# Two units pulled ahead of the first pairs, eight staging places, a table in six transfers, and a last tile that is written by tokens

## The reference, cut to what matters

```python
X = np.fft.rfft(x, axis=1)                       # x: 4 x 3008 x 256
Yr, Yi = Xr @ w_r - Xi @ w_i + b_r, Xr @ w_i + Xi @ w_r + b_i
Yr = np.sign(Yr) * np.maximum(np.abs(Yr) - 0.01, 0.0)   # Yi likewise
y = np.fft.irfft(Yr + 1j * Yi, n=3008, axis=1)
h = y.reshape(12032, 256) @ w_in                 # 256 x 2048
g = np.maximum(h, 0.0) + alpha * np.minimum(h, 0.0)
out = g @ w_out                                  # 2048 x 256
```

## Time and profile before

| | |
|---|---|
| median of 3 runs | 1375.19 us (1373.89 to 1375.62) |
| the profiled execution | 1378.68 us, of which the span is 1376.9 us |
| PE busy | 1360.3 us of the span (99%) |
| PEld, DVE, ACT, POOL busy | 84%, 75%, 55%, 24% |
| granted clock over the whole span | 0.996 |

### The profile page before, as it was taken

The page is one execution under the profiler, slowest core; times in us unless marked ns, Lnnn a source line. Parts: engine busy times, 40 slices in busy tenths (PEclk is TensorE's granted clock), DMA queues, the critical chain, the costliest instruction groups (busy, mean ns, idle before and its releaser), DMA issues.

```text
span 1376.9 us, 21744 instructions
## 1 busy us (share of the span) xinstructions
PE 1360.3 (99%) x6933; PEld 1158.1 (84%) x6933; DVE 1026.8 (75%) x1892; ACT 763.7 (55%) x1711; POOL 327.9 (24%) x370
## 2 busy tenths in 40 slices
PE   8999999999999999999999999999999999999997
PEld 5998888888888888888888888888888888888886
DVE  7787788898866768989866668888886566566654
ACT  4776566666544555756644446666564444444443
POOL 4534542232201422323300332233220000000000
PEclk9999999999999999999999999999999999999999
DMA  8554523231211541323312333223211021102101
GB/s 264 168 173 139 173 68 92 70 92 54 52 44 46 144 117 58 86 70 83 78 30 50 87 108 84 72 74 81 85 43 44 26 50 39 25 26 50 27 15 16
DMA packets 174896, 106.82 MB, mean 78 GB/s; under 512 B 112442, under 2 KB 150586, under 8 KB 174783
## 3 DMA queue, kind: packets, MB, share of 16 engines
q1 hardware_dynamic: 170344, 101.58, 27.4%
q10 hardware_dynamic: 3959, 3.70, 0.8%
q0 software_dynamic: 480, 0.16, 0.1%
HBM read 67.89 MB, written 37.49 MB: 77 GB/s over the span
## 4 chain that ended last, share of the span: by engine, by line
PE 93%; DVE 2%; ACT 2%; issue 1%; POOL 1%; DMA 1%; SPq 0%; POOLq 0%; ACTq 0%; DVEq 0%
PE out_ps L546 39%; PE h_ps L546 38%; PE work_ps L546 10%; PE work_ps L657 2%; PE work_ps L589 2%; PE work_ps L659 1%; ACT above L895 1%; PE work_ps L590 1%; DVE shrunk L1135 1%; POOL rows L1391 0%; SPq L381 0%; ACT shr_hi L901 0%; DMA rows<-in_idft_dram 0%; DMA rows<-in_x_dram 0%; DVE biased L1127 0%
## 5 line engine op out<-in xcount | busy, mean ns | idle before, releaser
L934 ACT ACTIVATE rows<-h_ps 128x502 f32<-128x502 f32 (+1 forms) x384 | 225.3, 587 | 510.3 <-PE h_ps L546 510.3
L1166 DVE SCALAR_TENSOR_TENSOR g_raw<-rows,keep,h_ps 128x502 f32<-128x502 f32 (+1 forms) x384 | 280.3, 732 | 264.6 <-ACT rows L934 261.3
L546 PE MATMUL out_ps<-g_hi,wout_hi 128*128 128x502 f32 (+1 forms) x768 | 305.0, 397 | 0.2
L546 PE MATMUL h_ps<-y_hi,win_hi 128*128 128x502 f32 (+1 forms) x768 | 300.0, 391 | 1.2 <-DVE g_raw L1166 1.0
L546 PE MATMUL out_ps<-g_hi,wout_lo 128*128 128x502 f32 (+1 forms) x768 | 299.8, 390 | 0.0
L546 PE MATMUL h_ps<-y_lo,win_hi 128*128 128x502 f32 (+1 forms) x768 | 299.7, 390 | 0.0
L546 PE MATMUL out_ps<-g_lo,wout_hi 128*128 128x502 f32 (+1 forms) x768 | 299.0, 389 | 0.0
L546 PE MATMUL h_ps<-y_hi,win_lo 128*128 128x502 f32 (+1 forms) x768 | 298.9, 389 | 0.0
L1065 DVE TENSOR_TENSOR g_lo<-g_raw,g_hi 128x502 fp32r<-128x502 f32 (+1 forms) x384 | 268.4, 699 | 1.8 <-ACT g_hi L943 1.4
L943 ACT ACTIVATE g_hi<-g_raw 128x502 fp32r<-128x502 f32 (+1 forms) x384 | 237.0, 617 | 6.7 <-DVE g_raw L1166 6.2
L546 PEld LDWEIGHTS h_ps<-y_hi,win_hi 128*128 128x128 f32 x768 | 145.0, 189 | 32.1 <-issue 2.0
(11 more groups left out here) (177 smaller groups left out, 2032.2 us busy)
## 6 DMA issues: line engine op xcount, KB each, us to landing
pair_raw<-fwd_scratch SPq DMA_DIRECT2D x96, 128.0 KB, 2.2
rows<-inv_scratch SPq DMA_DIRECT2D x61, 192.0 KB, 2.4
table<-in_twiddles_dram SPq DMA_DIRECT2D x28, 384.0 KB, 3.5
inv_scratch<-inv_sb SPq DMA_DIRECT2D x36, 256.0 KB, 2.2
x_raw<-in_x_dram SPq DMA_DIRECT2D x56, 160.0 KB
fwd_scratch<-staging SPq DMA_DIRECT2D x46, 192.0 KB, 2.1
inv_sb<-inv_scratch SPq DMA_DIRECT2D x122, 64.0 KB, 2.3
out_dram<-turned SPq DMA_DIRECT2D x124, 40.0 KB, 1.8
```

Of the source, the lines that this page charges most:

```text
L546: mm = pe.matmul(ps, lhs, rhs, start=(first and n == 0), stop=(last and n == len(terms) - 1), **kw)
L934: act.activation(negpart[:, q % 2, 0:size], h_ps[:, q % 2, 0:size], ACT.Relu, scale=-1.0).then_inc(negpart_done, 1)
L1166: dve.scalar_tensor_tensor(g_raw[:, q % 2, 0:size], negpart[:, q % 2, 0:size], keep[:, m:m + 1], h_ps[:, q % 2, 0:size], ALU.mult, ALU.add ...
```

## The change

It has four parts.

- **Units 16 and 17 come first** (`S_GAP` = 2). Their x is loaded by SP ahead of the first pairs, ACT makes the high part and DVE the rest after `mixw_lo`. PE runs 21 idle matmuls, unit 16, three idle ones, then the first pairs, with unit 17 where three idle matmuls stood. Four more (18 to 21) run behind the pairs, so that `S_EARLY` is 22 and tile 0 has none in steps 5 and 6. The idle matmuls now read `filler`, a part of `win_hi` set to ones. SP stores 16 and 17 inside the pair loop. DVE splits 18 and 19 in rounds 18 and 20 of the loop in place of rounds 19 and 21 for two units. `split_tw` goes ahead of `split_pair` and `split_shrunk` on ACT. `hidden(0, 0)` and `hidden(0, 1)` are in another order.
- **Eight places** for the rows of the head units (`above` and `inv_sb` are added).
- **The table in six transfers** of eight rows, not twelve of four.
- **The last tile's output by tokens**: `output_last` makes g the stationary operand in four blocks of 124 or 126 tokens, with tokens on partitions, 12 matmuls of 256 columns a step. DVE and ACT copy two blocks each, and twelve transfers of whole rows of 1 KB go out (seven on SP, three on ACT, two on POOL).

```diff
-S_LATE = 4
+S_GAP, S_LATE = 2, 6
-OUT_FIRST = 6
+OUT_FIRST = 8
+LAST_AT = (0, 124, 250, 376, 500)
+LAST_BLOCKS = len(LAST_AT) - 1
+        filler = win_hi[:, CHUNKS - 1, :, :].rearrange("p h f -> p (h f)")
             k = out_place(s)
             if k >= OUT_HEAD:
-                return (biased, shrunk)[k - OUT_HEAD][0:ROWS, :, :].rearrange("p q d -> p (q d)")
+                return (biased, shrunk, above, inv_sb)[k - OUT_HEAD][0:ROWS, 0:2, :].rearrange("p q d -> p (q d)")
...
 # SP
+            for s in range(S_HEAD, S_HEAD + S_GAP):
+                load_x(s)
             for p in range(4):
                 load_pair(p)
...
+                if k in (1, 3):
+                    store_fwd(sp, S_HEAD + k // 2)
                 if k in (5, 7, 9, 11):
-                    load_x(S_HEAD + (k - 5) // 2)
+                    load_x(S_HEAD + S_GAP + (k - 5) // 2)
...
-            for n in (0, 2, 4, 6):
-                store_out(sp, TILES - 1, n)
+            for n in (0, 1, 2, 4, 6, 8, 7):
+                store_last(sp, n, last_stored)
 # PE
+            def output_last(m):
+
+                q = (TILES - 1) * STEPS + m
+                pe.wait_ge(g_hi_done, q + 1)
+                for j in range(LAST_BLOCKS):
+                    at = slice(LAST_AT[j], LAST_AT[j + 1])
+                    ps = last_bank(j)[0:LAST_AT[j + 1] - LAST_AT[j], :]
+                    gh, gl = g_hi[:, q % 3, at], g_lo[:, q % 3, at]
+                    hi, lo = wout_hi[:, m // 2, m % 2, :], wout_lo[:, m // 2, m % 2, :]
...
+                    product(ps, [(gh, hi), (gh, lo)], first=m == 0, last=False)
+                    if j == 0:
+                        pe.wait_ge(g_lo_done, q + 1)
+                    mm = product(ps, [(gl, hi)], first=False, last=m == STEPS - 1)
...
-            stay_warm_early(29, h_ps[:, 1, :])
+            stay_warm_early(21, h_ps[:, 1, :])
+            forward1(S_HEAD)
+            stay_warm_early(3, h_ps[:, 1, :])
             for k in range(-1, PAIRS - 1):
                 forward2(k + 1)
                 if k == 0:
-                    stay_warm_early(3, out_ps[:, 1, :])
+                    forward1(S_HEAD + 1)
...
-            forward1(S_HEAD)
+            forward1(S_HEAD + 2)
             inverse2(PAIRS - 2)
-            forward1(S_HEAD + 1)
-            stay_warm(1)
+            forward1(S_HEAD + 3)
             inverse2(PAIRS - 1)
-            for u in (0, 2, 3, 4):
+            forward1(S_HEAD + 4)
+            for u in (0, 2, 3, 4, 1):
                 last_part(PAIRS - 2, u)
-            forward1(S_HEAD + 2)
-            last_part(PAIRS - 2, 1)
...
-            inverse1(0)
-            inverse1(2)
-            forward1(S_HEAD + 3)
-            inverse1(4)
-            inverse1(1)
+            for u in (0, 2, 4, 1):
+                inverse1(u)
+            hidden(0, 0, (0,))
             inverse1(3)
-            hidden(0, 0, (0,))
             inverse1(5)
-            hidden(0, 1, (0,))
+            forward1(S_HEAD + 5)
             hidden(0, 0, (1,))
-            hidden(0, 1, (1,))
+            hidden(0, 1)
 # ACT
+            for s in range(S_HEAD, S_HEAD + S_GAP):
+                x_arrived(act, s)
+                act.wait_ge(fwd_mm, s - 1)
+                act.activation(x_hi[0:NA, s % 2, :], x_place(s), ACT.Copy).then_inc(x_hi_done, 1)
             for p in range(2):
                 split_pair(p)
+            copy_fwd(S_HEAD)
             for k in range(-1, PAIRS - 1):
...
+                if k == 0:
+                    copy_fwd(S_HEAD + 1)
                 if k >= 1:
                     find_above(k - 1)
+                if k >= 0 and k % 3 == 0 and k // 3 + 1 < GROUPS:
+                    split_tw(k // 3 + 1)
                 if 2 <= k + 3 < PAIRS:
                     split_pair(k + 3)
                 if k >= 1:
                     split_shrunk(k - 1)
-                if k >= 0 and k % 3 == 0 and k // 3 + 1 < GROUPS:
-                    split_tw(k // 3 + 1)
...
+            for j in range(1, LAST_BLOCKS, 2):
...
+                act.activation(last_place(j)[rows_of, :], last_bank(j)[rows_of, :], ACT.Copy).then_inc(last_odd, 1)
+            for n in (10, 9, 11):
+                store_last(act, n, last_stored)
 # DVE
+            for s in range(S_HEAD, S_HEAD + S_GAP):
+                rest_x(s)
             for p in range(2):
                 rest_pair(p)
...
-                if k in (19, 21):
-                    split_x(S_HEAD + (k - 19) // 2, True)
+                if k in (18, 20):
+                    split_x(S_HEAD + S_GAP + (k - 18) // 2, True)
 # POOL
-            for e in range(PAIRS_END):
-                for b in range(2 * HEAD_V):
-                    load_last(e, b)
+            for b in range(2 * HEAD_V):
+                load_last(b)
```

More of the change, by code:

```diff
@@ L489, in _ @@
                     store_inv(k - 2)
-            for s in range(S_HEAD, S_EARLY):
+            for s in range(S_HEAD + S_GAP, S_EARLY):
                 store_fwd(sp, s)
-            for s in range(S_HEAD + 1, S_EARLY):
+            for s in range(S_HEAD + S_GAP, S_EARLY):
                 load_x(s + X_RING)
```

106 lines of the change are left out of this document (70 added, 36 removed).

## The result

The changed kernel takes 1380.59 us (median of 6 runs, 1378.84 to 1382.68), against 1375.08 of the kernel before beside it: ratio 1.0034, interval 1.0024 to 1.0044. It is 5.5 us slower where I forecast 10 us faster, and outside the range.

A forecast was written before the change was run, and what follows sets the result against it. PE, busy 99% of the span, was taken as the bound. Terms -1.4, -3.1, -1.8, -0.7, -1.4, +1.0 and -2.6 summed to -10.0 us, from 1375.19 to 1365.2 us; range 1362.5 to 1369.3.

The forecast's parts named there:

- The pair loop: From `forward2(3)` to the last mixing: an earlier twiddle split on ACT covers weight-load waits, 1.8 us less.
- Rival 2: Pair loop keeps its idle time, the wait only moving to the shrinking between DVE and ACT: 1367.0 us, 13 in 100.
- The first pairs: From `forward2(0)` to `forward2(3)`: 5.5 us of work at full clock plus 0.2 of waits, 3.1 us less.
- rival 1: PE stands 2 us at the start, the clock falls anyway and the first pairs gain nothing: 1368.3 us, 16 in 100.
- The start: First pair at 30.5 us, not 31.90, through an earlier table, fewer idle matmuls and earlier stores: 1.4 us less.
- rival 3: Loads of x undo the start: stores no earlier, `forward2(0)` at 31.9, clock falls: 1369.7 us, 5 in 100.
- Behind the loop: Between pair loop and `hidden(0, 2)`: one idle matmul fewer and a shorter wait for g, 0.7 us less.
- Tile 0: Two units at 0.70 us taken out of a PE without idle time there: 1.4 us less.
- The last tile: Its 16 steps each 0.065 us longer with 12 matmuls of 256 columns and hidden weight loads: 1.0 us more.
- the end: Behind the last `g_lo`: shorter copies, issues and landing, 6.4 us against 9.08, less 0.1: 2.6 us less.
- Rival 4: Last tile's weight loads come into the open, 14.5 us in place of 1.0: 1378.7 us, slower, 4 in 100.

The follow-up runs named there:

- 13: Kernel before with the twiddle split ahead on ACT, and POOL's part of it waiting until DVE's `shr_lo` is done: 1376.07 us, ratio 0.9999.
- 1: Changed kernel with ACT's twiddle split moved back behind the shrunk high part in the pair loop: 1377.60 us, ratio 1.0016.
- 8: Kernel before with only the twiddle split moved ahead of `split_pair` and `split_shrunk` on ACT: 1379.59 us, ratio 1.0031.
- 5: Changed kernel with the twiddle split moved back and SP's store of unit 21 behind the loads of back pair 3: 1375.04 us, ratio 0.9992.
- 6: Kernel of 5 with 30 idle matmuls ahead of unit 16, not 21, and x split in rounds 19 and 21, not 18 and 20: 1371.79 us.
- 11: Kernel before with 37 idle matmuls ahead of pair 0 in place of 29: 1375.01 us, ratio 0.9991.
- 2: Changed kernel with SP's store of unit 21 and the x load of unit 25 moved behind the loads of back pair 3: 1376.66 us.
- 4: Changed kernel with 32 idle matmuls ahead of unit 16 in place of 21: 1380.82 us, ratio 1.0039.
- 7: Kernel before with only the table in six transfers and eight places for the head's rows: 1374.24 us, ratio 0.9990.
- 9: Kernel before with the table in six transfers, eight places and the last tile's output by tokens: 1372.09 us, ratio 0.9969.
- 12: Kernel of 9 with DVE's split of x of unit 17 moved from round 21 to behind the shrinking of pair 22: 1372.72 us.
- 15: Kernel of 9 with the twiddle split ahead on ACT and POOL's part of it behind `shr_lo`: 1372.45 us, ratio 0.9977.
- 10: Kernel of 6 with x of units 16 and 17 loaded behind the first pairs and tables, and the units run in rounds 2 and 3: 1377.15 us.
- kernel 3: Kernel before with only the last tile's output by tokens: 1374.30 us, ratio 0.9984.
- 14: Kernel of 6 with the twiddle split ahead of `split_pair` on ACT and POOL's part waiting for `shr_lo`: 1373.07 us, ratio 0.9985.

## Why the prediction was wrong, by its own steps

**The pair loop (-1.8, came +4.6): the step that failed.** I wrote that `split_tw` "0.9 us earlier on ACT covers waits of at most 0.7", and priced the other side at 0.5 us of ACT's time that PE needs "a round later". The price of ACT was not the loss: with ACT's order as moved, the loop is 0.24 us longer (13). What failed is that I moved an instruction on ACT and did not ask where its successor on POOL would then lie. It lies beside `pair_lo` and `shr_lo`, which take 1.04 and 1.23 us and end about 0.3 us after POOL's instruction does. The split moved back gives 3.5 of the 4.6 us (1), alone on the kernel before the same edit costs 4.0 (8), and with POOL held back 0.24 (13). Of the remaining 1.1 most comes from the splits of x in rounds 18 and 20, for which I left 0.6; moved to 19 and 21 they cost 0.9 less (5 against 6). Rival 2 named the place, a wait moved to the shrinking, but as lost gain and not as a loss. The Trainium skill ("SBUF — State Buffer", two separate sides) has the rule: DVE and GpSimd share one pair of ports as an exclusive lock, which a DVE instruction with two SBUF inputs needs against a GpSimd instruction that reads SBUF, and the loser blocks for the whole instruction. The trace agrees: `pair_lo`, `shr_lo` and `x_lo`, with two SBUF inputs, are held, and `biased` and `spec_lo`, which read PSUM, take 0.42 us in the mean in 8 and 13, with POOL's split beside them or not. The runs show who is held and for how long; that it is a lock on ports is the page's account of it. I had not weighed it.

**The first pairs (-3.1, came -0.4).** Two things were wrong. The clock fell in the profiled execution, so rival 1 came true there: unit 16 was 1.6 us later than forecast and PE stood 3.00 us in one piece. But the term was also no gain to be had off the median. I said that the profiled execution lay 3.5 us above the median and took its differences off the median all the same. That 3.5 was in the main this very fall of the clock: without it the same stretch is 3.2 us shorter (11), and by the mean clocks 9 of 115 executions of the kernel before have the whole of it, 42 a part and 64 none. The unit 17 in place of idle matmuls and waits is free, as forecast: 5.55 us to `forward2(3)` at full clock in 2 and 4, 5.63 in 11.

**The start (-1.4, came +0.4).** The table and the places are worth more than I said, 2.3 us in one trace (7) and 1.8 in the mean. The rest of the part takes it away, much as rival 3 had it. With unit 16 ahead of the pairs, pair 0 begins at 31.2 to 32.5 us (seven traces), without it at 29.5 to 29.9 (7, 9, 12, 15). The two loads of x stand ahead of stores and pair loads in transfers that are full (0.98 from 5 to 23 us), and the pair loads go out at 27.5 to 29.4 with them and at 26.4 to 27.0 without. For the landing of the table's last transfer I had 4.9 us and 0.4 more. It took 6.8, but 5.8 in 7 and 6.3 in 9 with no load of x in the way, so the larger part of what I missed comes without x. On DVE the first rest of x is held beside POOL's `itw_lo`: 2.08 us for the two rests, not 1.40, by the effect that I missed in the pair loop. How the delay is shared between full queues and DVE was not measured apart; 10 took both away and had 30.24.

**Behind the loop (-0.7, came -0.4).** Right in kind; the wait before `hidden(0, 2)` is 0.32 as forecast.

**Tile 0 (-1.4, came +1.7).** I said that PE has no idle time there and looked at PE alone. The units taken out do give 1.0 us (2, 6). But the last early unit is now copied later, SP waits for it, and the loads of back pair 3 are queued behind. The step not taken was to list what stands behind the moved store in SP's order.

**The last tile (+1.0, came +0.8) and the end (-2.6, came -3.1)** were right in mechanism and near in size, and kernel 3 shows the net alone. The 2.0 us to land had no row behind it; the two transfers for which the trace has a landing, both issued by POOL, took 2.3 and 2.4, near the fixed cost that I cited, which the page of the Trainium skill has in its section on a transfer issued by POOL and not under Specifications. Rival 4 did not come: the steps take 2.76 us with 12 matmuls, pitch 0.118, and each weight load hidden. The rule of the Trainium skill ("TensorE: Matmul & The Clock Gate", Part 3) that I set beside the row, that only loads into another row group overlap, isn't what this kernel shows. In rival 4 I put the limit at 0.174 us a matmul; 11.0 us over 16 steps is 0.171.

**The sum of the medians.** The spans differ by 3.7, the medians by 5.5. The rest is again which executions were profiled: the one before 3.6 above its median, the one after 2.1 above.

**A kernel that beats both.** 6 (ratio 0.9974) and 9 (0.9969) are 3.6 and 4.3 us under the kernel before; between them the measurement does not decide. Part of that is the clock: one of their 14 executions has a mean clock of 0.997 and the others 0.999 or 1.000.

**What stays open.** When the clock falls. PE stood 2.60 us before unit 16 and it held (2), stood 2.57 in the same place and it fell (1: 0.59 from 32 to 39 us), stood 0.23 and it fell (5, 14). Kernels whose PE stands 0.6 us or less at the start keep it there in their profiled executions (6, 7, 9, 11, 12, 15), but so do some that stand for 1.31 and 1.73 us (13, 8), and no rule that decides a single case came out. The Trainium skill ("TensorE: Matmul & The Clock Gate", Part 1) says that the number of matmuls at the lower level at a kernel's start differs from run to run of one kernel; the mean clocks of the 115 executions, 0.996 to 0.999, agree in kind.

## What to carry to other kernels

When an instruction moves, follow its result to the next engine: ask what that engine's instruction will lie beside, above all where POOL and DVE both read two SBUF operands, and which issues are queued behind any store that must wait for it. Before a profiled execution's differences are taken off a median, account for how far it stands above that median; what makes it stand there can't be won twice. Early loads into a full stretch of transfers can delay whatever is queued behind them, even if the engine that wants them has time to spare.

## What the hardware showed that I had not expected

- A DVE subtraction of two SBUF operands of 128x256 takes 0.42 us, and 1.04 or 1.23 beside a POOL subtraction of 128x384, ending some 0.3 us behind it; one with a PSUM operand is not held (0.415 to 0.421 us in the mean in 8 and 13).
- A transfer of eight rows of the table, 2.9 KB, issued at 18.12 landed 6.83 us later, where the queues had carried 324 GB/s from 5 to 23 us.
- In closely related kernels the granted clock fell to 1.2 GHz at the start (before), at 106 us (5, 14), at 125 us (4) or not at all (2, 6), and a fall cost between 1.5 us (4: eight matmuls at 0.42 us, not 0.23) and 3.2 (before). With the same start it fell for the whole stretch, for a part of it (3) or not at all (8, 13).
